# A row of inverse roots in device memory, kept in the order of partitions and read with a step

## The reference

```python
x = local_attention(q, k, v)             # window of 64, 32 heads in all; out (2304, 512)
rms = sqrt(mean(x * x, axis=-1, keepdims=True) + 1e-6)
xn = x / rms * rms_g                     # what the change touches
g = xn @ w_gate                          # (512, 1536)
y = (silu(g) * (xn @ w_val)) @ w_out     # (2304, 512)
r = maximum(y @ w_in, 0)                 # (512, 2048)
out = (r * r) @ w_out2                   # (2304, 512)
```

## Time and profile before

| | |
|---|---|
| median of 3 runs | 870.01 us (869.5 to 870.76) |
| profiled execution | 869.6 us |
| its span in the trace | 867.8 us |
| granted TensorE clock | 0.998 |
| TensorE busy | 851.2 us, 98% |
| VectorE busy | 588.8 us, 68% |
| ACT busy | 477.2 us, 55% |
| GpSimd busy | 468.0 us, 54% |

### The profile page before, as it was taken

The page is one execution under the profiler, slowest core; times in us unless marked ns, Lnnn a source line. Parts: engine busy times, 40 slices in busy tenths (PEclk is TensorE's granted clock), DMA queues, the critical chain, the costliest instruction groups (busy, mean ns, idle before and its releaser), DMA issues.

```text
span 867.8 us, 16812 instructions
## 1 busy us (share of the span) xinstructions
PE 851.2 (98%) x6390; PEld 839.5 (97%) x6390; DVE 588.8 (68%) x729; ACT 477.2 (55%) x1001; POOL 468.0 (54%) x471
## 2 busy tenths in 40 slices
PE   7898999999999999999999999999999999999998
PEld 6787999999999999999999999999999999999998
DVE  4668776468557558755557767678677777677982
ACT  6787566545565645555554455554455454555451
POOL 4656398493589665388857368222187212386100
PEclk9999999999999999999999999999999999999999
DMA  8773122322222232222222322256622266523587
GB/s 300 246 225 88 49 74 74 64 77 61 82 72 73 74 73 61 79 74 74 73 56 61 85 68 74 55 164 225 218 86 71 71 222 185 169 73 98 179 254 246
DMA packets 109871, 100.98 MB, mean 116 GB/s; under 512 B 8544, under 2 KB 87520, under 8 KB 109792
## 3 DMA queue, kind: packets, MB, share of 16 engines
q1 hardware_dynamic: 92544, 84.04, 32.8%
q10 hardware_dynamic: 17248, 15.87, 5.5%
HBM read 80.48 MB, written 19.40 MB: 115 GB/s over the span
## 4 chain that ended last, share of the span: by engine, by line
PE 91%; DVE 3%; issue 2%; ACT 2%; POOL 1%; DVEq 0%; POOLq 0%; ACTq 0%
PE banks L840 29%; PE banks L841 29%; PE banks L842 29%; ACT probs L1165 1%; PE banks L810 1%; DVE probsT L1498 1%; PE banks L751 1%; PE banks L824 1%; PE banks L784 1%; DVE acts L1438 0%; DVE banks L1478 0%; PE banks L759 0%; POOL h L689 0%; POOL d_lo L696 0%; DVE xc_lo L1629 0%
## 5 line engine op out<-in xcount | busy, mean ns | idle before, releaser
L840 PE MATMUL banks<-xc_hi,w_hi 128*128 128x384 f32 x844 | 282.5, 335 | 0.2 <-DVE xc_lo L1470 0.2
L842 PE MATMUL banks<-xc_hi,w_lo 128*128 128x384 f32 x844 | 281.9, 334 | 0.0
L841 PE MATMUL banks<-xc_lo,w_hi 128*128 128x384 f32 x844 | 281.9, 334 | 0.0
L840 PE MATMUL banks<-hs_hi,d_hi 128*128 128x384 f32 x544 | 182.3, 335 | 0.8 <-POOL d_lo L696 0.6
L842 PE MATMUL banks<-hs_hi,d_lo 128*128 128x384 f32 x544 | 181.7, 334 | 0.0
L841 PE MATMUL banks<-hs_lo,d_hi 128*128 128x384 f32 x544 | 181.7, 334 | 0.0
L840 PEld LDWEIGHTS banks<-xc_hi,w_hi 128*128 128x128 f32 x844 | 158.4, 188 | 0.6 <-DVE xc_lo L1470 0.4
L841 PEld LDWEIGHTS banks<-xc_lo,w_hi 128*128 128x128 f32 x844 | 158.4, 188 | 0.0
L842 PEld LDWEIGHTS banks<-xc_hi,w_lo 128*128 128x128 f32 x844 | 158.4, 188 | 0.0
L1414 DVE TENSOR_TENSOR w_lo<-w_raw,w_hi 128x1024 fp32r<-128x1024 f32 x58 | 75.6, 1303 | 82.1 <-ACT w_hi L1086 81.8
L578 POOL TENSOR_TENSOR w_raw<-w_raw 128x256 f32<-128x256 f32 x58 | 61.8, 1065 | 122.1 <-DVE d_lo L1584 52.2
(11 more groups left out here) (115 smaller groups left out, 1333.7 us busy)
## 6 DMA issues: line engine op xcount, KB each, us to landing
w_kept<-stash SPq DMA_DIRECT2D x56, 256.0 KB, 3.2
w_raw<-in_w_gate SPq DMA_DIRECT2D x36, 256.0 KB, 2.9
w_raw<-in_w_val SPq DMA_DIRECT2D x72, 128.0 KB, 2.9
d_raw<-in_w_out SPq DMA_DIRECT2D x36, 256.0 KB, 2.6
d_raw<-in_w_down SPq DMA_DIRECT2D x32, 256.0 KB, 2.9
v_sb<-in_v_rows SPq DMA_DIRECT2D x16, 384.0 KB, 4.3
w_raw<-in_w_in SPq DMA_DIRECT2D x24, 256.0 KB, 2.7
w_raw<-in_w_in SPq DMA_DIRECT2D x48, 128.0 KB, 2.6
```

The lines of the kernel that those rows point to most:

```text
L840: pe.matmul(ps, w_h, v_h, start=first, stop=False, skip_group_check=joined)
L841: pe.matmul(ps, w_h, v_l, start=False, stop=False, skip_group_check=joined)
L842: return pe.matmul(ps, w_l, v_h, start=False, stop=last, skip_group_check=joined)
```

## The change

The row in device memory changes its order. Before, token n*128 + p stood at place n*128 + p of the row, so that the six numbers of a partition lay 512 bytes apart. Now it stands at place p*6 + n: the six numbers of one partition lie together, and the row is no longer in the order of tokens. The load is the same instruction. The products that apply the row read it with a step of six numbers, through a view (n, p) of the loaded tile; their other operands keep their order, written as six runs of 128. No instruction is added or removed.

```diff
+        def by_block(t):
+            return t.rearrange("p (n t) -> p n t", n=TB)
...
             def rinv_store(q):
 
                 act.wait_ge(rinv_done, q + 1)
-                act.dma_start(rinv_rows[q, :].rearrange("(n p) -> p n", p=P), rms[:], allow_slow_non_contiguous=True).then_inc(rows_out, 16)
+                act.dma_start(rinv_rows[q, :].rearrange("(p n) -> p n", p=P), rms[:]).then_inc(rows_out, 16)
...
                             if f in (1, 2, 3, 4):
                                 dve.wait_ge(rb_in, 16 * q)
-                                normalise(pair_cols(q, f - 1), f - 1, rb[:])
+                                normalise(by_block(pair_cols(q, f - 1)), f - 1, rb[:].rearrange("p (t n) -> p n t", n=TB))
```

## The result

The changed kernel takes 873.88 us (median of 6 runs, 872.67 to 874.31) beside 870.11 us for the kernel before (6 runs); the ratio is 1.0043, 95% interval 1.003 to 1.0056. It is slower by 3.8 us; forecast were 875.0 us and slower. The profiled execution has a span of 872.6 us.

What follows compares the result with a forecast made beforehand. TensorE bounds the kernel, busy 851.2 of 867.8 us. First wait -1.6, second wait 0, stops for `d_lo` +6.6 gave +5.0: 874.6 us profiled, 875.0 against the median; range 868.1 to 877.0.

Steps and rivals of the forecast that it cites:

- The store: Ends of token blocks 0 and 1: 128 runs land in 1.8 to 4.4 us; ACT's wait goes, gaining 1.63 us, then nothing.
- The price of a product: Eight VectorE products reading the row with a step of six: +0.8 us each, a second pass, ends 0 and 0.96.
- The row of 6 numbers from PSUM: VectorE's `mean_square`: 7.5 ns more for 6 numbers 256 bytes apart, giving 0.96 us over 768 as upper price.
- the rival built on it: The step is free: eight products stay at 2 us, only the first wait is seen, 868.4 us; chance 0.33.
- The room: Four down chunks per place: VectorE and GpSimd take turns reading SBUF, filling 4.2 of 4.16 us despite VectorE's 1.23 idle.
- The size of the stops: TensorE waiting for GpSimd's `d_lo` in both places: 3.3 us each, between 2.4 and 4.2, so 6.6 us.
- The walk through the turns: Four down chunks at +0.8 us: TensorE stops 1.65 us, later 1.7; with refilling 3.6 us at one place.
- the bookkeeping: Smaller step prices, four products a place: at 0.5 us, 4 x 0.5 - 0.85 = 1.15 us a place.
- the slack of 0.85 us: Down chunks: GpSimd's `d_lo` is ready about 0.85 us before TensorE's next chunk must have it.
- the rival of a partial price: The step costs a part, 0.3 to 0.6 us a product: 2.3 for both places, less 1.6, 870.7 us; chance 0.07.

Runs made afterwards that it cites:

- the test products: Kernel before with 128x768 products behind VectorE's last instruction, nothing of GpSimd beside: 1.01 and 1.02 us dense, 1.58 each for the last four, stepped on various operands.
- the one-input maximum: Kernel before with a VectorE maximum over 128x512 of one SBUF tile added ahead of each of the eight products: ratio 0.9992.
- the second trace of the changed kernel: Changed kernel as it is, timed again for comparison on one chip: 873.59 us, ratio 1.0041.
- the addition: Kernel before with a VectorE addition of 128x512 from two SBUF tiles added ahead of each of the eight products: ratio 1.0022.
- step of three: Changed kernel with the products reading the row with a step of 3 numbers, not 6; tokens get other tokens' roots: ratio 1.0003.
- step of six in halves: Changed kernel with each stepped product as two of 128x384: median 871.8 us, ratio 1.001.
- the trace with the longest landing: Profile of the kernel with the old store and stepped products; its slow store took 12.4 us to land: 875.85 us, ratio 1.0054.

## Why the prediction was right, point by point

**The store.** Right. The wait on ACT goes in both places, place 1 falls by 140.3 - 138.7 = 1.6 us as worked out, place 2 by nothing. The landing of 2.2 to 3.2 us lies in the range given. That the same gain was to be had without the new order, by a sooner store, the prediction didn't see.

**The price of a product.** Right in kind, a little large. I took +0.8 us between 0 and 0.96; it is +0.67 in place (1.48 less 0.81) and +0.56 to 0.57 with nothing beside (1.58 to 1.59 less 1.02). The row of 6 numbers from PSUM pointed the right way and was too dear by a third or more (0.96). No run shows that a step in PSUM and one in SBUF have one cause, and the price is not a whole second pass either (0.56 us on top of 1.02). That 0.8 came so near is in part luck. The Trainium skill (SBUF — State Buffer, section on the DMA port swizzle) says that four fp32 numbers are the furthest free stride, with lines of 16 bytes; the test products agree that the full price is reached where each number is in a line of its own, but a step of three numbers already costs 0.23 us and a step of four, free by the page, costs it all. The Trainium skill (VectorE: DVE Perf Modes, section on Mode 1×) describes the fp32 mode as one result a cycle that makes no assumptions on strides. Taken as a price this doesn't hold here (1.58 us against 1.02): the rival built on it, 868.4 us, needed products unchanged at 2.0 us.

**The room.** The mechanism was right: TensorE waits for `d_lo` and for nothing else, GpSimd's first sum takes 2.14 us beside the 2.2 forecast, and without GpSimd's sums the same products cost nothing. VectorE's idle time of 1.23 us a chunk, which a busy table shows as room, was none for a two-input instruction, and was room for the one-input maximum.

**The size of the stops.** Forecast 3.3 us a place, measured 2.5 and 2.6: 5.1 and not 6.6. This is the term that was mis-sized. The walk through the turns had a first stop of 1.65 us, and it is there (1.53 in place 1, 1.04 in place 2; 1.53 and 1.54 in the second trace of the changed kernel). It had the same again two chunks later, 1.7 us. What came was a stop of 0.30 us one chunk later, and in place 2 one of 0.41 three chunks later. A product was also 0.13 us cheaper than assumed; its share and that of the order of turns are not separated by a run. In the other direction, the walk counts the refilling of 0.27 us once where two stops have it twice, so its own terms make 3.9 us and not 3.6. With the 1.6 us won, +5.0 was forecast; it is +3.6 in the two places (0.9 and 2.7), and +3.8 in the medians.

**What failed in it** is the bookkeeping by which I priced the smaller cases: added time times four, less the slack of 0.85 us. With the own times of the traces it compares as follows, in us a place (for the addition place 2):

| added to each of four chunks | own time added | by the bookkeeping | measured |
|---|---|---|---|
| step of three | 0.24 | 0.1 | 0.9 |
| step of six | 0.67 | 1.8 | 2.5 and 2.6 |
| addition, an instruction more | 0.55 | 1.35 | 1.0 |
| step of six in halves, an instruction more | 0.71 | 2.0 | 1.4 |

One longer product costs 0.7 to 0.8 us a place more than the bookkeeping has, and a second instruction in each chunk costs less than it has. So the rival of a partial price, 870.7, was priced too low. This fits the order of turns: a waiting instruction gets the next turn whole, so a single long product pushes `d_lo` past its due time, while two instructions let GpSimd in between. The halves show this for the changed kernel itself, 1.001 against 1.0041. Why the slack covers next to nothing at a step of three I read from one row; a run that moves `d_lo` against the product wasn't made.

## What to carry to other kernels

Before you make a transfer cheaper, look whether it can be issued sooner: here one moved line gave all that a new order in memory could (0.9969 beside 0.9967). A layout that helps a transfer is paid by each instruction that reads it; read it once, on an engine with room (ACT here), and keep the repeated readers dense. And an engine's idle time is room only for instructions that don't share anything: look who is waiting while it runs, and how long the single instruction is.

## What the runs showed of the hardware that was not expected

A step of four or more fp32 numbers costs a 128x768 operation 0.55 to 0.62 us on VectorE (1.57 to 1.64 against 1.02) and 0.72 us on ACT (1.56 against 0.84). On VectorE, at a step of six, it costs that once, however many operands are stepped; a step of two is free on VectorE and costs 0.08 us on ACT. The landing of the same 3 KB store in 768 pieces varied from 9.4 to 12.4 us, and what TensorE lost by the first one from 1.0 to 2.3 us. In the trace with the longest landing, two stops of TensorE of 1.33 and 0.44 us were followed by some 3.4 us at the lower clock, which cost 1.7 us more; a single stop of 1.53 us in the changed kernel was followed by none (granted clock 1.00 in 190:192).
